# Phi in two buffers and made a pair ahead, VectorE's small steps placed among the maxima

## What is computed

```python
scores = where(causal, -1e9, scale * q @ k.T)
a = exp(scores - max); a /= a.sum(-1) + 1e-9
local = a @ v
phi(x) = where(x > 0, x, exp(x) - 1) + 1
mem_out = phi(q) @ M_prev / (phi(q) @ z_prev + 1e-6)
attn = g * mem_out + (1 - g) * local          # g = sigmoid(beta), per head
x = attn, heads side by side
x = piecewise(x @ w_in) @ w_out               # first feed-forward layer
out = silu(x @ w_in2) @ w_out2                # second
```

## Time and profile before

| what | us |
|---|---|
| median of three runs (lowest, highest) | 1141.76 (1140.83, 1142.0) |
| the profiled execution, its own time | 1140.68 |
| its span in the trace | 1138.9 |
| PE, DVE, ACT, POOL busy in the span | 1043.7, 482.0, 412.8, 260.6 |

### The profile page before, as it was taken

How to read it: one execution, slowest core, us unless ns; L and a number is a source line. 1 busy time by engine, 2 the same in 40 slices (tenths; PEclk the granted TensorE clock), 3 DMA queues, 4 the chain that set the end, 5 groups by cost and what they waited for, 6 DMA issues and landing times.

```text
span 1138.9 us, 16400 instructions
## 1 busy us (share of the span) xinstructions
PE 1043.7 (92%) x6256; PEld 951.7 (84%) x6256; DVE 482.0 (42%) x1063; ACT 412.8 (36%) x935; POOL 260.6 (23%) x276
## 2 busy tenths in 40 slices
PE   5778686877779999999999999999999999999998
PEld 4556565656569999999999999999999999999997
DVE  6464655546345444444444444432332323233222
ACT  4545454555523233332323335532322323222222
POOL 5554636465578000000000006610000000000000
PEclk8888888888889999999999999999999999999999
DMA  5333333323123000000000004400000000000000
GB/s 159 98 96 100 99 89 110 88 88 89 45 65 93 20 1 1 1 0 0 0 0 1 1 11 127 133 1 1 28 1 28 0 18 9 0 28 1 28 1 28
DMA packets 30204, 48.02 MB, mean 42 GB/s; under 512 B 3264, under 2 KB 13504, under 8 KB 30144
## 3 DMA queue, kind: packets, MB, share of 16 engines
q1 hardware_dynamic: 27584, 38.81, 11.6%
q0 software_dynamic: 2560, 8.39, 2.4%
HBM read 42.47 MB, written 4.72 MB: 41 GB/s over the span
## 4 chain that ended last, share of the span: by engine, by line
PE 81%; POOL 6%; DVE 5%; ACT 3%; issue 2%; DMA 1%; SPq 0%; DVEq 0%; ACTq 0%; POOLq 0%
PE ps L903 24%; PE ps L902 24%; PE ps L901 23%; PE ps L777 3%; PE ps L796 3%; POOL phir L313 2%; POOL phir L311 2%; POOL phie L316 2%; PE ps L845 2%; PE ps L821 1%; DVE mden L587 1%; PE ps L784 1%; ACT phir L393 1%; ACT turned L434 1%; DVE probT L624 1%
## 5 line engine op out<-in xcount | busy, mean ns | idle before, releaser
L901 PE MATMUL ps<-xhi,W 128*128 128x384 f32 x768 | 258.8, 337 | 5.2 <-DVE xlo L693 5.2
L903 PE MATMUL ps<-xhi,W 128*128 128x384 f32 x768 | 258.7, 337 | 0.0
L902 PE MATMUL ps<-xlo,W 128*128 128x384 f32 x768 | 258.3, 336 | 0.0
L713 DVE TENSOR_TENSOR glo<-act_t,ghi 128x384 fp32r<-128x384 f32 x192 | 111.1, 579 | 221.2 <-ACT ghi L491 221.2
L491 ACT CAST ghi<-act_t 128x384 fp32r<-128x384 f32 x192 | 98.7, 514 | 230.5 <-PE ps L903 211.5
L296 POOL TENSOR_TENSOR W<-stage,W 128x512 fp32r<-128x512 f32 x64 | 83.1, 1308 | 331.5 <-ACT W L533 328.4
L901 PEld LDWEIGHTS ps<-xhi,W 128*128 128x128 f32 x768 | 145.1, 189 | 9.4 <-issue 5.3
L902 PEld LDWEIGHTS ps<-xlo,W 128*128 128x128 f32 x768 | 145.0, 189 | 4.1
L903 PEld LDWEIGHTS ps<-xhi,W 128*128 128x128 f32 x768 | 145.0, 189 | 0.0
L796 PE MATMUL ps<-ident,prob 128*128 128x128 f32 x320 | 67.2, 366 | 71.0 <-DVE probT L624 68.4
L901 PE MATMUL ps<-ghi,W 128*128 128x384 f32 x384 | 128.3, 334 | 0.0
(11 more groups left out here) (109 smaller groups left out, 1425.2 us busy)
## 6 DMA issues: line engine op xcount, KB each, us to landing
qraw<-in_qT SPq DMA_DIRECT2D x16, 320.0 KB, 3.0
vn<-in_vN SPq DMA_DIRECT2D x16, 320.0 KB, 2.9
kraw<-in_kT SPq DMA_DIRECT2D x16, 288.0 KB, 2.8
qn<-in_qN SPq DMA_DIRECT2D x16, 288.0 KB, 4.5
zb<-in_zN SPq DMA_DIRECT2D x32, 144.0 KB, 3.1
out_x<-ostage SPq DMA_DIRECT2D x18, 256.0 KB, 2.0
stage<-in_moe_w_in POOLq DMA_DIRECT2D x16, 256.0 KB, 3.9
stage<-in_moe_w_out POOLq DMA_DIRECT2D x16, 256.0 KB, 3.5
```

Source lines behind the costliest of these rows:

```text
L713: nc.vector.tensor_tensor(glo[:, f % SLOTS, :], a, ghi[:, f % SLOTS, :].bitcast(F32), ALU.subtract).then_inc(glo_done, 1)
L901: nc.tensor.matmul(dst, w_lo_, x_hi_, start=first, stop=False)
L902: nc.tensor.matmul(dst, w_hi_, x_lo_, start=False, stop=False)
L903: return nc.tensor.matmul(dst, w_hi_, x_hi_, start=False, stop=last)
```

## The change

`phie` and `phir` get two buffers, by the parity of the pair. On ACT the two phi activations of pair p + 1 move from the end of iteration p to behind its first copy, and `exps(p + 1, 5)` moves ahead of the copy of T_REST. On DVE the order of one iteration is written anew: `to_x(p - 1)` first, the steps of `rows` and `norms` between other work, the copy of T_M31 ahead of `maximum(p + 1, 3)`, `low_k` and `low_q` two maxima earlier. The orders of PE, POOL and SP stay as they were.

```diff
--- before.py
+++ after.py
@@ -66,8 +66,8 @@
         qhi = [sb(f"qhi{i}", [P, MAIN + P], F32R, where=att) for i in range(2)]
         qlo = [sb(f"qlo{i}", [P, MAIN + P], F32R, where=att) for i in range(2)]
         qn = sb("qn", [P, NB, D], where=att)
-        phie = sb("phie", [P, NB, D], where=att)
-        phir = sb("phir", [P, NB, D], where=att)
+        phie = [sb(f"phie{i}", [P, NB, D], where=att) for i in range(2)]
+        phir = [sb(f"phir{i}", [P, NB, D], where=att) for i in range(2)]
         zb = sb("zb", [P, NB, D], where=att)
         phs = sb("phs", [P, NB + 1, D], where=att)
         vn = sb("vn", [P, 2, FULL + 1, 2, D], where=att)
@@ -308,12 +308,13 @@
 
             def phi_whole(p):
                 pool.wait_ge(phi_part, 2 * p + 2)
-                nc.gpsimd.tensor_tensor(phir[:], qn[:], phir[:], ALU.add).then_inc(phi_sum, 1)
+                both, e = phir[p % 2], phie[p % 2]
+                nc.gpsimd.tensor_tensor(both[:], qn[:], both[:], ALU.add).then_inc(phi_sum, 1)
                 pool.wait_ge(phi_sum, 2 * p + 1)
-                nc.gpsimd.tensor_tensor(phir[:], phir[:], phie[:], ALU.add).then_inc(phi_sum, 1)
+                nc.gpsimd.tensor_tensor(both[:], both[:], e[:], ALU.add).then_inc(phi_sum, 1)
                 pool.wait_ge(phi_sum, 2 * p + 2)
                 pool.wait_ge(z_in, 32 * (p + 1))
-                nc.gpsimd.tensor_tensor(phie[:], phir[:], zb[:], ALU.mult).then_inc(phi_norm, 1)
+                nc.gpsimd.tensor_tensor(e[:], both[:], zb[:], ALU.mult).then_inc(phi_norm, 1)
 
             def weigh_v(p):
                 pool.wait_ge(v_in[p % 2], 16 * (p // 2 + 1))
@@ -328,10 +329,10 @@
                 pool.wait_ge(row_step, 4 * p + 4)
                 if p:
                     pool.wait_ge(t_full, TURNS * (p - 1) + T_REST + 1)
-                nc.gpsimd.tensor_tensor(phs[:, 0:2 * FULL, :], phir[:, 0:2 * FULL, :],
+                nc.gpsimd.tensor_tensor(phs[:, 0:2 * FULL, :], phir[p % 2][:, 0:2 * FULL, :],
                                         rw[:, 1, 0:2 * FULL].unsqueeze(2).broadcast_to([P, 2 * FULL, D]),
                                         ALU.mult).then_inc(weighed, 1)
-                nc.gpsimd.tensor_tensor(phs[:, 2 * FULL:, :], phir[:, 2 * FULL:, :].broadcast_to([P, 2, D]),
+                nc.gpsimd.tensor_tensor(phs[:, 2 * FULL:, :], phir[p % 2][:, 2 * FULL:, :].broadcast_to([P, 2, D]),
                                         rwt[:, 1, :].unsqueeze(2).broadcast_to([P, 2, D]),
                                         ALU.mult).then_inc(weighed, 1)
 
@@ -388,15 +389,15 @@
 
             def phi_part_1(p):
                 act.wait_ge(n_in, 16 * (p + 1))
-                if p:
-                    act.wait_ge(weighed, 2 * p)
-                nc.scalar.activation(phir[:], qn[:], ACT.Relu, scale=-1.0).then_inc(phi_part, 1)
+                if p >= 2:
+                    act.wait_ge(weighed, 2 * p - 2)
+                nc.scalar.activation(phir[p % 2][:], qn[:], ACT.Relu, scale=-1.0).then_inc(phi_part, 1)
 
             def phi_part_2(p):
                 act.wait_ge(phi_part, 2 * p + 1)
-                if p:
-                    act.wait_ge(norm_step, 4 * p - 3)
-                nc.scalar.activation(phie[:], phir[:], ACT.Exp, scale=-1.0).then_inc(phi_part, 1)
+                if p >= 2:
+                    act.wait_ge(norm_step, 4 * p - 7)
+                nc.scalar.activation(phie[p % 2][:], phir[p % 2][:], ACT.Exp, scale=-1.0).then_inc(phi_part, 1)
 
             def exps(p, c):
                 act.wait_ge(s_read, NB * p + c + 1)
@@ -446,6 +447,9 @@
             for p in range(NPAIR):
                 more = p + 1 < NPAIR
                 empty_first(p)
+                if more:
+                    phi_part_1(p + 1)
+                    phi_part_2(p + 1)
                 empty_main(p, T_M20, 2, 0)
                 if more:
                     exps(p + 1, 0)
@@ -458,12 +462,11 @@
                 if more:
                     exps(p + 1, 4)
                 empty_phi(p)
+                if more:
+                    exps(p + 1, 5)
                 empty_rest(p)
                 empty_row(p)
                 if more:
-                    phi_part_1(p + 1)
-                    exps(p + 1, 5)
-                    phi_part_2(p + 1)
                     exps(p + 1, 6)
                     exps(p + 1, 7)
                     exps(p + 1, 8)
@@ -584,7 +587,7 @@
             def norms(p, step):
                 if step == 0:
                     dve.wait_ge(phi_norm, p + 1)
-                    nc.vector.tensor_reduce(mden[:, 0], phie[:], AX.X, ALU.add).then_inc(norm_step, 1)
+                    nc.vector.tensor_reduce(mden[:, 0], phie[p % 2][:], AX.X, ALU.add).then_inc(norm_step, 1)
                     return
                 dve.wait_ge(norm_step, 4 * p + step)
                 if step == 1:
@@ -651,37 +654,37 @@
             dve.wait_ge(made, 12)
             for p in range(NPAIR):
                 more, more2 = p + 1 < NPAIR, p + 2 < NPAIR
-                rows(p, 0)
                 if p:
                     to_x(p - 1)
+                rows(p, 0)
+                empty_second(p)
                 rows(p, 1)
-                empty_second(p)
+                if more:
+                    maximum(p + 1, 0)
                 rows(p, 2)
                 if more:
-                    maximum(p + 1, 0)
+                    maximum(p + 1, 1)
                 rows(p, 3)
-                if more:
-                    maximum(p + 1, 1)
                 empty_main(p, T_M21, 2, 1)
                 if more:
                     maximum(p + 1, 2)
+                empty_main(p, T_M31, 3, 1)
+                if more:
                     maximum(p + 1, 3)
-                empty_main(p, T_M31, 3, 1)
+                if more2:
+                    low_k(p + 2)
                 if more:
                     maximum(p + 1, 4)
                     maximum(p + 1, 5)
                 if more2:
-                    low_k(p + 2)
+                    low_q(p + 2)
                 if more:
                     maximum(p + 1, 6)
+                    norms(p + 1, 0)
                     maximum(p + 1, 7)
-                if more2:
-                    low_q(p + 2)
-                if more:
-                    maximum(p + 1, 8)
-                    norms(p + 1, 0)
                     norms(p + 1, 1)
                     norms(p + 1, 2)
+                    maximum(p + 1, 8)
                     norms(p + 1, 3)
             to_x(NPAIR - 1)
```

## The result

| kernel | median us | lowest to highest | ratio to before, 95% interval |
|---|---|---|---|
| before | 1141.34 | 1140.83 to 1142.0 | |
| changed | 1155.67 | 1154.97 to 1159.52 | 1.0131, 1.0114 to 1.0149 |

The changed kernel is 14.3 us slower. The forecast was 1154. The attention ends 16.1 us later: the last write of X starts at 341.12, against 325.06 before.

The account below looks back on a forecast made before the run. Attention was taken as bound by a ring of waits through phi, POOL's steps and T_M1's copy. Fourteen pairs add 13.4 us, the ends -1.5: +11.9 on 1140.68, plus 1.08 to the median, so 1154; range 1143 to 1168.

Parts of the forecast that it names:

- Which wait comes next: In attention, PE's 4.24 us wait for DVE's copy of T_M1 goes; ACT waits for the load of `qn` instead, 5 us a pair.
- The landing and the way to PE: `qn` lands 6.0 us after the pair's start; after two phi activations and T_M20's copies PE resumes at +8.0.
- the estimate of +4.8: `qn` landing 4.8 us after the pair's start, from a one-transfer fit giving 2.7 us for 288 KB; the prediction rejected it.
- The tail's start: The tail's turn in a pair starts at +12.64 us, against +12.11 before: 0.53 later.
- From the tail to the next pair: After the tail's start, same order; 0.86 us more of PE's work at half clock speed costs 0.43 us a pair.
- VectorE's order: DVE's copy of T_M31 ahead of the third maximum delays score 3 by 0.13 us a pair; small steps cost nothing.
- The rival with this mechanism: DVE's `low_k`, ahead of maxima 4 and 5, waits a whole POOL step: 0.9 us a pair, 1166 us; chance 0.13.
- the small steps' saving: DVE's small steps in `rows` and `norms` leave PE's waiting path, but PE waits for ACT there, so the load covers it.
- The two ends: Pair 0's tail comes 4.4 us later; pair 15 gains 4.6 plus 1.3 for the clock; together -1.5 us.
- The other side's price: Rival: `qn` is in time, 68.4 us of PE's waits for T_M1's copy go, 1073 us or less; chance 0.06.

## Why the prediction was right, by its steps

**Which wait comes next.** Right. The wait moved from DVE's copy of T_M1 to the load of `qn`, over ACT's copies of T_M20, in 15 pairs. The load put first, and phi asked for later, show the cause from both ends.

**The landing and the way to PE.** Forecast +6.0 and +8.0; measured +6.03 and +8.02 in pair 6, and 5.64 to 6.70, in the mean 6.17, for the start of ACT with `qn` over pairs 1 to 14. The program's start was the right row to go by. `qn` landed 3.9 us (median) after its own issue, with v, m and z just ahead of it, 3.6 with v alone ahead, and the same 288 KB of k in 2.8. The fit in the Trainium skill, page "DMA: Bandwidth & Descriptors", section "Anatomy of one DMA — SWDGE (gpsimd) path", is for one transfer, and the estimate of +4.8 worked out from it is not what a transfer in a row of four showed.

**The tail's start.** Forecast +12.64. The mean over pairs 1 to 14 is +12.68. Before it was +11.93 on the mean; I took the 12.11 of pair 7 for it, so the difference is 0.75 and not 0.53.

**From the tail to the next pair.** I added 0.43 for the clock, for a low stretch that would end 2.16 us beyond the tail's start. The mean did grow by 0.41, from 7.76 to 8.17 (mean pairs 19.68 and 20.85 over pairs 1 to 14, less the tails). But this step was wrong, and that its figure came out is luck. The low stretch was as long as before in most pairs, but it began in the stall, and in pair 6 it was over at the tail's start. Worked out from PEclk in each pair, the lower level takes 0.49 us of this part of a pair in the kernel before, and 0.62 in the changed one, over half of it in pair 11 alone; in pairs 5 to 10 and 12 to 14 it takes none. At half speed that is 0.06 us of growth. The other 0.35 is VectorE's new order. Pair 9 has the clock at 1.00 in this part in both kernels; before:

```profile
202.91:210.42 7.51, 7.27 (x78) 5.76 (x76) 3.28 (x8) 5.51 (x14) 1.15 (x1) 1.00 0.32 86
```

and changed, with score 4 in it:

```profile
217.76:226.19 8.43, 7.53 (x78) 5.79 (x77) 5.49 (x16) 5.30 (x14) 5.18 (x6) 1.00 0.37 107
```

```profile
219.08 0.30 PE L784 MATMUL ps<-khi,qlo 128*128 128x64 f32 x1 [0.66 <-DVE negmax L584]
```

With VectorE's old order this part takes 8.06 (mean pair 20.51, tail 12.44), and there the clock is the reason as I had thought: the lower level takes 1.19 us of it, worth 0.35 more than before.

**VectorE's order.** I gave it 0.13 us a pair, for the third maximum. The run with the old order puts it at 5.6 us in all, 0.35 to 0.4 a pair. The term was mis-sized, because I let `klo` ahead of maxima 4 and 5 pass as free unless POOL held it up. POOL did hold it up: `klo` took 1.54 us in place of 0.75, to 155.6, beside POOL's step of 153.57 with 1.42, and score 4 then waited. But its place counts for more than its length. With the load first `klo` took 0.75 us ahead of these maxima, and moving it behind them still gave 7.4 us; with the old order it took 1.46, and 1.04 with the load first besides, and from 60 to 210 us PE does not wait at score 4 in either. The rival with this mechanism was right in kind; on its price, 0.9 a pair, it was too high in all, though pair 9 shows such a pair. I also wrote that the small steps' saving was covered by the load. Uncovered, it proved to be nothing.

**The two ends.** Pair 1 begins 5.5 us later than before (forecast 4.4): the tail of pair 0 comes 4.4 later as forecast, and 1.1 is added behind it at a clock of 1.00, 0.82 of it a wait of score 4 for DVE's maximum. Pair 15 takes 5.7 less (forecast 5.9), of which 5.4 lie before its tail (forecast 4.6) and 0.3 behind it (forecast 1.3). The fourteen pairs between add 16.3 (forecast 13.4). Together 16.1 of attention against 11.9; 0.8 of it is not in the span's growth of 15.3.

**The other side's price.** For a load in time I wrote 1073 or less, which counts the waits alone; it was 1055.85 with the load moved and 1075.66 with phi moved. The clock, for which I gave nothing, comes on top: PE's busy time in a pair is 15.51 before and 12.91 with the load first, at a clock of 1.00.

## What to carry to other kernels

When a step is moved ahead, look at when its input is asked for by the queue that loads it. A load that sits behind another's wait for a buffer is as late as that buffer, and it shows in no wait as long as its user is later still. A moved use and its load belong in one edit: here the change without the load's line cost 14 us, the line without the change gave nothing, and both together gave 85.

A stall on the busiest engine costs more than its length, and taking it away gives back more. And an order of small steps on an engine that "has room" should be tried once the larger wait is gone; two of the moves here cost 10 us, where the whole order had cost 5.6 behind the load's wait.

## What the runs showed of the hardware

TensorE's granted clock followed the stall. With a stall of 5.35 us in the pair its mean is 0.83, with one of 3.23 us (the load of `qn` between v and m) 0.90, and with waits of 0.4 us 1.00. PE's busy time for the same instructions is 14.84, 14.00 and 12.91 us. The clock had fallen some 2.3 us before the stall of 5.35 us ended, so a part of the low stretch cost nothing.

A DVE step on two operands in SBUF (`klo`) took 1.54 us where POOL's step of 1.42 us had begun 0.5 us before it, and 0.75 where it began 0.01 us before POOL's step; that POOL step then took 2.02 us in place of 1.40. In the first case the next POOL step, which began while `klo` still ran, took 1.78 in place of 1.25. I had counted on DVE's delay and not on POOL's: the two engines hold each other up in turn.
